# Three-stage order for attention pairs, mask in VectorE's maximum pass, features off GpSimd

## What is computed

```python
B, H, S, D = 4, 8, 576, 64
scores = q @ k.T / 8                      # causal: -1e9 above the diagonal
a = exp(scores - max) ; a /= a.sum + 1e-9
local = a @ v
phi(x) = where(x > 0, x, exp(x) - 1) + 1
mem_out = (phi(q) @ M_prev) / (phi(q) @ z_prev + 1e-6)
g = sigmoid(beta)                         # one per head
x = g * mem_out + (1 - g) * local         # 2304 tokens x 512
# first layer: h = x @ w_in (512 -> 1024); u = h * softmax(h); layer norm with g_ln; @ w_out
# second layer: (sigmoid(x @ w_gate) * (x @ w_val)) @ w_out, width 1536
```

## Time and profile before

| | us |
|---|---|
| median of 3 runs | 964.6 (963.66 to 966.36) |
| profiled execution | 962.04 |
| its span | 960.3 |
| busy PE, DVE, ACT, POOL | 907.2, 408.5, 329.8, 183.5 |
| mean granted TensorE clock | 0.979 |

### The profile page before, as it was taken

How to read it: one execution, slowest core, us unless ns; L and a number is a source line. 1 busy time by engine, 2 the same in 40 slices (tenths; PEclk the granted TensorE clock), 3 DMA queues, 4 the chain that set the end, 5 groups by cost and what they waited for, 6 DMA issues and landing times.

```text
span 960.3 us, 15231 instructions
## 1 busy us (share of the span) xinstructions
PE 907.2 (94%) x5584; PEld 749.3 (78%) x5584; DVE 408.5 (43%) x972; ACT 329.8 (34%) x740; POOL 183.5 (19%) x144
## 2 busy tenths in 40 slices
PE   5787789999999999999799999999999999999997
PEld 2555557777777777878699989989998998998997
DVE  5666776666766676354414422122112112112112
ACT  3455545545554555345524211121112112112111
POOL 4344322222222120125407410010001001001000
PEclk9889999999999999999999999999999999999999
DMA  5131111111111100400305000000000000000000
GB/s 155 49 127 41 51 40 38 31 33 38 38 38 38 38 26 14 132 1 1 99 1 165 0 33 1 1 18 15 0 0 33 0 0 33 0 0 33 0 0 33
DMA packets 36786, 33.51 MB, mean 35 GB/s; under 512 B 5776, under 2 KB 27280, under 8 KB 36752
## 3 DMA queue, kind: packets, MB, share of 16 engines
q1 hardware_dynamic: 36752, 33.06, 11.6%
HBM read 28.33 MB, written 4.72 MB: 34 GB/s over the span
## 4 chain that ended last, share of the span: by engine, by line
PE 87%; DVE 5%; issue 2%; POOL 2%; ACT 1%; DMA 1%; POOLq 0%; ACTq 0%; SPq 0%; DVEq 0%
PE m_bk L1066 8%; PE s_bk L1089 6%; PE tt_bk L1174 5%; PE s_bk L1176 5%; PE s_bk L1174 5%; PE s_bk L1175 5%; PE tt_bk L1176 5%; PE tt_bk L1175 5%; PE o_bk L1007 5%; PE tt_bk L999 4%; PE s_bk L953 4%; PE o_bk L1089 4%; PE m_bk L1191 3%; PE m_bk L1190 3%; PE m_bk L1189 3%; PE s_bk L1066 2%
## 5 line engine op out<-in xcount | busy, mean ns | idle before, releaser
L886 DVE TENSOR_TENSOR gv<-gv,s_bk 128x384 f32<-128x384 f32 x71 | 39.4, 554 | 289.4 <-PE s_bk L1176 289.4
L530 ACT ACTIVATE p_nat<-s_bk,negmax 128x512 f32<-128x512 f32 (+2 forms) x144 | 77.9, 548 | 94.9 <-DVE negmax L729 94.8
L597 ACT ACTIVATE gv<-tt_bk 128x384 f32<-128x384 f32 x70 | 34.5, 492 | 206.7 <-PE tt_bk L1176 206.7
L1174 PE MATMUL tt_bk<-x_hi,w_hi 128*128 128x384 f32 x280 | 94.7, 338 | 8.2 <-POOL x_lo L492 8.2
L1174 PE MATMUL s_bk<-x_hi,w_hi 128*128 128x384 f32 x288 | 96.3, 334 | 0.0
L1176 PE MATMUL s_bk<-x_hi,w_lo 128*128 128x384 f32 x288 | 96.2, 334 | 0.0
L1175 PE MATMUL s_bk<-x_lo,w_hi 128*128 128x384 f32 x288 | 96.2, 334 | 0.0
L1176 PE MATMUL tt_bk<-x_hi,w_lo 128*128 128x384 f32 x280 | 94.3, 337 | 0.0
L1175 PE MATMUL tt_bk<-x_lo,w_hi 128*128 128x384 f32 x280 | 94.0, 336 | 0.0
L604 ACT CAST gv_hi<-gv 128x384 fp32r<-128x384 f32 x72 | 36.9, 513 | 158.0 <-PE m_bk L1191 135.9
L729 DVE TENSOR_REDUCE negmax<-s_bk 128x1 f32<-128x512 f32 (+2 forms) x144 | 67.4, 515 | 51.0 <-PE s_bk L953 42.7
(11 more groups left out here) (144 smaller groups left out, 1846.6 us busy)
## 6 DMA issues: line engine op xcount, KB each, us to landing
qkT<-in_q SPq DMA_DIRECT2D x16, 288.0 KB, 2.8
qkT<-in_k SPq DMA_DIRECT2D x16, 288.0 KB, 2.8
out<-o_sb SPq DMA_DIRECT2D x18, 256.0 KB, 2.0
v_raw<-in_v SPq DMA_DIRECT2D x16, 256.0 KB, 2.7
w_raw<-in_moe_w_gate SPq DMA_DIRECT2D x12, 256.0 KB, 4.5
w_raw<-in_moe_w_val SPq DMA_DIRECT2D x12, 256.0 KB, 4.9
w_raw<-in_moe_w_out SPq DMA_DIRECT2D x12, 256.0 KB, 6.0
xT<-in_moe_w_in SPq DMA_DIRECT2D x1, 2048.0 KB, 8.5
```

What stands on the lines that cost most here:

```text
L530: nc.scalar.activation(dst, s_tile(tile), ACT.Exp, bias=negmax[:, n:n + 1], accum_out=den[:, n:n + 1]).then_inc(exp_ok, 1)
L1174: mm(o, w3_hi[f][:, a], x2_hi[:, d, :], start=d == 0, stop=False)
```

## The change

- A pair spreads over three steps: step g does the scores of g, memory and fills of g-1, and the weighting of g-2. `M0` becomes 6, there are 17 steps, and the last has no scores. No loop is left in this part.
- `p_nat` and the buffer of queries and keys exist twice. Loads of q and k are issued one step earlier, v and the memory rows follow in the later step.
- No mask products and no scaled queries. VectorE's maximum is one `tensor_tensor_reduce`: scores plus a float32 mask, times -1/8, written to `p_nat`, and the minimum of it as the negative maximum. ScalarE takes the exponential in place in `p_nat`.
- Score groups wait for `max_ok` and not for `exp_ok`.
- Features: relu and exp on ScalarE straight from q, and min(exp, 1) + relu on VectorE. GpSimd keeps the splits and the power.
- ScalarE copies fills 0, 2, 4, 5, 6, VectorE 1, 3.
- The tail of the weighted rows goes into a bank of its own (`tail_bank`, in `m_bk`), directly behind the main part.
- The tail scores stand late, among the output products. On ScalarE `moe_x(t + 1)` and `feature_exp(g + 1)` stand ahead of `moe_y(t - 1)`.
- The weights' splits move: W1 to steps 1 and 2, W2 to 4 and 5 (two blocks each) and 6 (four).

```diff
-    M0 = HP + 1
+    M0 = HP + 2
-    T_END = LAST - M0
+    T_END = PAIRS - M0
-        W1_AT = {0: (0, 1), 1: (2, 3)}
-        W2_AT = {2: (0, 1, 2), 3: (3, 4, 5), 4: (6, 7)}
+        W1_AT = {1: (0, 1), 2: (2, 3)}
+        W2_AT = {4: (0, 1), 5: (2, 3), 6: (4, 5, 6, 7)}
...
@@ gpsimd @@
+            def step(g):
+                for c in W1_AT.get(g, ()):
+                    split_w1(c)
+                for f in W2_AT.get(g, ()):
+                    split_w2(f)
+                if g >= M0:
+                    rstd(g - M0)
+                if g >= M0 - 1:
+                    split_x(g - M0 + 1)
...
@@ scalar @@
-                nc.scalar.activation(dst, s_tile(tile), ACT.Exp, bias=negmax[:, n:n + 1],
+                nc.scalar.activation(p_tile(g, tile), p_tile(g, tile), ACT.Exp, bias=negmax[:, n:n + 1], scale=-1.0,
                                      accum_out=den[:, n:n + 1]).then_inc(exp_ok, 1)
...
+            def step(g, t):
+                if g < PAIRS:
+                    exp_tile(g, 0)
+                    exp_tile(g, 1)
+                if t:
+                    moe_ln(t - 1)
+                keep_both(g - 2)
+                if g < PAIRS:
+                    for n in range(2, 8):
+                        exp_tile(g, n)
+                if g < LAST:
+                    feature_relu(g + 1)
+                keep_pt(g - 1, 0)
+                moe_exp(t)
+                keep_pt(g - 1, 2)
+                if g < PAIRS:
+                    exp_tile(g, 8)
+                keep_pt(g - 1, 4)
+                moe_square(t)
+                keep_pt(g - 1, 5)
+                keep_pt(g - 1, 6)
+                for f in W2_AT.get(g, ()):
+                    split_w2(f)
+                moe_x(t + 1, x_done(t + 1))
+                if g < LAST:
+                    feature_exp(g + 1)
+                if t:
+                    moe_y(t - 1)
...
@@ vector @@
-                    last = nc.vector.tensor_reduce(negmax[:, c:c + 1], s_tile(tile),
+                    last = nc.vector.tensor_tensor_reduce(out=to, in0=s_tile(tile), in1=m, scale=-SCALE, scalar=3.0e38,
+                                                          op0=ALU.add, op1=ALU.min, accum_out=negmax[:, c:c + 1])
...
+            def feature(g):
+                dve.wait_ge(qrelu_ok, g + 1)
+                dve.wait_ge(qexp_ok, g + 1)
+                wait(dve, mem_ready, 2 * g)
+                nc.vector.scalar_tensor_tensor(out=phi[:, 0:S], in0=qexp[:, :], scalar=1.0, in1=qrelu[:, :], op0=ALU.min,
+                                               op1=ALU.add).then_inc(phi_ok, 1)
...
+            def early_step(g):
                 unit_max(g, 0)
                 unit_max(g, 1)
+                if g:
+                    normalize(g - 1, 1)
+                    normalize(g - 1, 2)
                 unit_max(g, 2)
                 unit_max(g, 3)
+                if g:
+                    scale_memory(g - 1, 0)
+                    scale_memory(g - 1, 1)
+                    keep_pt(g - 1, 1)
                 unit_max(g, 4)
                 unit_max(g, 5)
+                if g:
+                    keep_pt(g - 1, 3)
+                feature(g)
                 unit_max(g, 6)
+                normalize(g, 0)
...
+            def step(g, t):
+                if g < PAIRS:
+                    unit_max(g, 0)
+                    unit_max(g, 1)
+                if t > 1:
+                    moe_store_x(t - 2)
+                normalize(g - 1, 1)
+                if t:
+                    moe_ln_low(t - 1)
+                normalize(g - 1, 2)
+                if g < PAIRS:
+                    unit_max(g, 2)
+                    unit_max(g, 3)
+                scale_memory(g - 1, 0)
+                scale_memory(g - 1, 1)
+                if g < PAIRS:
+                    feature(g)
+                    unit_max(g, 4)
+                    unit_max(g, 5)
+                    normalize(g, 0)
+                moe_max(t)
+                keep_pt(g - 1, 1)
+                moe_rows(t)
+                moe_stats(t)
+                keep_pt(g - 1, 3)
+                if g < PAIRS:
+                    unit_max(g, 6)
+                for f in W2_AT.get(g, ()):
+                    scale_w2(f)
+                moe_var(t)
+                moe_norm(t)
...
@@ tensor @@
+            def early_step(g):
                 scores(g, 0)
+                if g > 1:
+                    weighted(g - 2)
+                scores(g, 1)
+                if g:
+                    memory(g - 1, None)
+                scores(g, 2)
+                if g:
+                    for n in range(5):
+                        turn_p(g - 1, n)
+                scores(g, 3)
+                if g:
+                    turn_p(g - 1, 5)
+                    turn_p(g - 1, 6)
+
+            def step(g, t):
+                if g < PAIRS:
+                    scores(g, 0)
+                if t > 1:
+                    moe_out_t(t - 2)
+                if t:
+                    pe.wait_ge(pt_act_ok, NA * (g - 1))
+                    pe.wait_ge(pt_dve_ok, ND * (g - 1))
                     moe_transpose(t - 1)
+                weighted(g - 2)
+                wait(pe, yt_ok, t - 1)
+                if g < PAIRS:
+                    scores(g, 1)
+                memory(g - 1, t)
+                pe.wait_ge(x_ok, 2 * (g - 1))
+                wait(pe, u_ok, t)
+                moe_hidden(t, 0, 12)
+                if g < PAIRS:
+                    scores(g, 2)
+                moe_hidden(t, 12, 24)
+                turn_p(g - 1, 0)
+                turn_p(g - 1, 1)
+                if t:
+                    if g < PAIRS:
+                        pe.wait_ge(max_ok, NU * g + NU - 1)
+                    moe_out(t - 1, 0, 8)
+                turn_p(g - 1, 2)
+                turn_p(g - 1, 3)
+                if t:
+                    moe_out(t - 1, 8, 12)
+                if g < PAIRS:
+                    scores(g, 3)
+                if t:
+                    moe_out(t - 1, 12, 16)
+                turn_p(g - 1, 4)
+                turn_p(g - 1, 5)
+                if t:
+                    moe_out(t - 1, 16, 20)
+                turn_p(g - 1, 6)
+                if t:
+                    moe_out(t - 1, 20, 24)
```

More of the change, by code:

```diff
@@ L427, in feature_min @@
[L427 to L435, removed]
+            nc.gpsimd.affine_select(out=mask[:, (FULL - 1) * P:FULL * P], in_=mask[:, (FULL - 1) * P:FULL * P],
+                                    compare_op=ALU.is_ge, fill=MASK, base=0, pattern=[[-1, P]],
+                                    channel_multiplier=1).then_inc(mask_ok, 1)
@@ L454, in rstd, with step @@
                 nc.gpsimd.tensor_tensor(st[:, 6:7], st[:, 5:6], half[:, :], ALU.pow).then_inc(rstd_ok, 1)
[L456 to L483, removed]
+            def step(g):
+                for c in W1_AT.get(g, ()):
[6 more added lines that the diff above has]
+                    split_x(g - M0 + 1)
+            for g in range(PAIRS + 1):
+                step(g)
             def split_w3(f):
@@ L604, in keep_gv_hi, with keep_both @@
                 nc.scalar.copy(gv_hi[f % 2][:, :], gv[f % 2][:, :]).then_inc(gv_hi_ok, 1)
[L606 removed]
+            def keep_both(h):
+                keep_x(h, 0)
+                keep_x(h, 1)
+            def early_step(g):
                 exp_tile(g, 0)
                 exp_tile(g, 1)
[L610 to L619 removed]
+                if g > 1:
+                    keep_both(g - 2)
+                for n in range(2, 6):
+                    exp_tile(g, n)
+                if g:
+                    keep_pt(g - 1, 0)
+                    keep_pt(g - 1, 2)
@@ L866, in _ @@
             dve.wait_ge(gates, 2)
-            feature_relu(0)
             for g in range(M0):
-                step(g, early=W2_AT.get(g, ()))
-            step(M0, t=0, first=True, t_turned=False)
-            step(M0 + 1, t=1, t_turned=False)
-            with dve.Fori(M0 + 2, LAST) as g:
-                step(g, t=g - M0)
-            step(LAST, after=False, t=T_END)
+                early_step(g)
+            for g in range(M0, PAIRS + 1):
+                step(g, g - M0)
             t = T_END
@@ L971, in scores @@
                     for pair in zip(*units):
[L972 to L973 removed]
                         for tile, unit in zip(pair, units):
[L975 removed]
+                            last = score_tile(g, tile)
                             if tile == unit[-1]:
@@ L1138, in _ @@
+            pe.wait_ge(consts, 4)
             pe.wait_ge(zeros, 2)
             for g in range(M0):
-                step(g, before=g > 0)
-            step(M0, t=0, first=True)
-            step(M0 + 1, t=1, turned=False)
-            with pe.Fori(M0 + 2, LAST) as g:
-                step(g, t=g - M0)
-            step(LAST, t=T_END)
+                early_step(g)
+            for g in range(M0, PAIRS + 1):
+                step(g, g - M0)
             t = T_END
-            weighted_main(LAST)
+            weighted(LAST)
```

345 lines of the change are left out of this document (124 added, 221 removed).

## The result

The changed kernel takes 959.0 us (median of 6 runs, 956.3 to 960.6), the kernel before 964.3 us beside it. The ratio is 0.994, with a 95% interval of 0.992 to 0.996: faster, by 5.3 us, where 12.4 us were forecast. The profiled execution's span fell from 960.3 to 957.0 us, by 3.3 us only: the profiled execution of the kernel before lies 2.3 us under its median, that of the changed kernel 0.3 us.

What follows compares the result with a forecast made beforehand. Early steps were taken as held by waits for exponentials and transpose copies, full steps by TensorE's work. Terms of 91 + 55 + 205.1 + 22.1 = 373.2 against 385.6 gave -12.4 us: 952 on the runs' scale, range 939 to 965.

Steps and rivals of the forecast that it cites:

- rival B: Full steps: ScalarE's output copy comes in time, steps run at TensorE's 24.7 us, kernel 944 us; chance 0.17.
- The early steps: Attention-only steps before the first feed-forward tile: that tile's pair starts at 91 us instead of 107.4, a gain of 16.4.
- The walk of one round: Early steps, one tail maximum's end to the next, added up engine by engine: 14.2 us, 5.4 less than before.
- Splitting the layers' weights adds 1.3: Early steps: 1.3 us added to the four rounds' 56.8 us for splitting the layers' weights.
- The 2 us put down for the low clock: Early steps: 2 us added to the four rounds' sum for low-clock stretches.
- The transition: Steps 6 and 7: GpSimd's splits delay its power, TensorE idles some 8 us; both steps take 55 us against 49.2.
- Full steps, TensorE: Full steps: TensorE loses 0.74 us of mask products, leaving 24.7 us of work; moving groups costs nothing visible.
- Full steps, ScalarE: Full steps: the output copy stands last in ScalarE's queue, TensorE waits 0.9 us, a step takes 25.6 us.
- VectorE's edits: Masked maximum costs as before plus up to 0.08 us per tile; features' sum on VectorE costs 0.7 us.
- Rival D: VectorE becomes the bound: masked maximum takes twice the time per column, 3.3 us more per step, 971 us; chance 0.09.
- Rival C: Early steps hardly shrink: waits for memory, transposes and copies plus low clock, rounds 16.8 us, kernel 965; chance 0.17.
- A: The prediction's own sum for the whole kernel: 952 us, alone 945 to 959; chance 0.57.

Runs made afterwards that it cites:

- e5: Changed kernel with GpSimd's four passes over the first weights held back until VectorE's fourth unit of maxima of the next step; 949.4 us (ratio 0.985).
- e8: Changed kernel with the edits of e3, e4 and e5, holding back both weights' splits, low part of x ahead of them; 933.8 us (ratio 0.969).
- e3: Changed kernel with GpSimd's power of a tile issued ahead of the splits of the second weights in step 6; 951.4 us (ratio 0.987).
- e1: Changed kernel with the low parts of the first weights subtracted on VectorE, not on GpSimd; 953.8 us (ratio 0.990).
- e2: Changed kernel with each of GpSimd's four 1024-column passes over the first weights cut into four of 256 columns; 954.4 us (ratio 0.991).
- e6: Changed kernel with two more GpSimd passes in step 4, into buffers that nothing reads; 963.6 us in one run.
- e4: Changed kernel with ScalarE's copy of the layer's output ahead of the next tile's copy and the features' exponential; 952.4 us (ratio 0.988).
- e7: Kernel before with the mask part alone: no mask products, masks in VectorE's maximum pass, exponential from SBUF, full-step loop written out; 953.8 us (ratio 0.990).

## Why the prediction was right and wrong

The direction and the range held; the size did not. 12.4 us were forecast, 5.3 came (3.3 by the two profiled executions, which the table compares). By stretches:

| | forecast | measured | |
|---|---|---|---|
| start of step 6 | 91 | 103.9 | +12.9 |
| steps 6 and 7 | 55 | 55.95 | +1.0 |
| full steps, eight | 8 x 25.6 | 8 x 25.05 | -4.7 |
| step 16 | 22.1 | 21.6 | -0.5 |
| behind the pairs | 574.7 | 575.2 | +0.5 |

That the range held is in part luck: 5 us that the later steps took less than forecast hid part of the 12.9 us of the early ones. Two sums are slightly off: eight steps of 25.6 us are 204.8 and not 205.1, and rival B with early rounds at 13.5 us gives some 941 and not 939. Neither changes the outcome.

**The early steps: the step that failed.** The walk of one round was nearly right: 14.2 us forecast, 14.70 measured in step 4, and 15.0 in step 1 against 15.5. What failed is the term "Splitting the layers' weights adds 1.3". The text gives no working and no row for it, and in the whole walk of the early steps GpSimd's passes have no price: work on an engine that nobody waits for was put at nothing, without a reason. Measured against step 4, step 2 is 4.85 us longer, step 3 6.8 and step 5 2.9, 14.5 us together, where the terms for the splits and the low clock had 3.3. VectorE standing beside GpSimd's passes is 10.3 of the 14.5; the rest goes with the lower clock of these steps. When e5 and e8 moved GpSimd's passes, 13.1 of the 14.5 went: 10.2 in steps 2 and 3, and 2.9 in step 5. The split between the steps differs from execution to execution. From tail maximum to tail maximum, steps 2 and 3 take 19.6 and 21.0 us here, and 20.6 and 20.7 in e3, whose edit does not touch them.

e1, e2, e5 and e6 show the cause: a GpSimd pass with its inputs in SBUF, and a VectorE scaling in SBUF or a pass with two SBUF inputs, exclude each other, whole instruction by whole instruction. The Trainium skill, SBUF — State Buffer, section Who interferes with whom, states this rule: a VectorE pass in a two-port mode, or one with two SBUF inputs against a GpSimd pass that reads SBUF, and the GpSimd pass block each other for the whole instruction. The traces agree: 2.39 us for a scaling and 2.32 for the pass over three numbers in the changed kernel, and in e3 an unchanged 0.69 for the 512-column maximum, which has only one input in SBUF. That the scalings run in a two-port mode is not shown by a run here.

GpSimd's work was not new. New is that the change moved nine scalings from the middle and the end of a step to its start, where GpSimd begins as soon as ScalarE has given it the high parts. In the order before, at this place stood maxima out of PSUM and one relu. That relu carries the mark. By the same count VectorE stood for 4.0 us in all five early steps of the kernel before. The row of the relu:

```profile
L737 DVE TENSOR_SCALAR qrelu<-qkT x16: 445/451/1864, 6.7 to 337.8; 128x576 f32<-128x576 f32 x16
```

A pass that takes 0.45 us took up to 1.86. That one ran from 29.32 to 31.18 us, beside two splits of 2.4 and 2.6 us. Had the walk charged the full length of such splits, the term would have been near 5 us per step.

The 2 us put down for the low clock were about right for what is left when the exclusion is gone (1.4 in step 3 of e5). In the changed kernel step 3 has 2 us more than step 2 at a mean clock of 0.76 against 0.83, and e1, without the exclusion, has two equal steps at 0.90. Whether the stall lets the clock fall stays open. The clock is also low without any stall: 0.89 in step 4 of e1 and of e4, which takes 15.9 us there. And step 6 of the changed kernel keeps 1.00 although VectorE stood for 2.8 us in it, with more products for TensorE in that step.

**The transition.** Forecast some 8 us of idle time before the transposes of step 7, measured 8.37, with the chain as described; without it the step takes 27.5 us (e3). This came from reading the order of one short queue line by line.

**Full steps, TensorE.** 24.7 us of work forecast, 24.24 measured. The mask products were sized right. Missing were the 0.17 of the products that now run as one group (e7), and some 0.25 for the new order, which the text called "nothing visible": both without masks and without waits, a full step takes 24.55 us in the old order (e7) and 24.30 in the new one (e4). That fewer changes between kinds of products are the reason is not shown.

**Full steps, ScalarE.** A wait of 0.9 us was forecast, with its cause, and 0.81 measured. e4 took it away by the order of three instructions. Rival B, full steps of 24.7 us because the copy comes in time, did not come: the wait was there, and the step's 25.05 us lie near 24.7 only because TensorE's own work was less than forecast.

**VectorE's edits.** The maximum with mask costs what the maximum cost, 0.68 us for 512 columns. The first line is the kernel before, the others the changed one:

```profile
L729 DVE TENSOR_REDUCE negmax<-s_bk 128x1 f32<-128x512 f32 x16 | 10.3, 686 | 5.9 <-PE s_bk L953 5.9
...
L719 DVE CUSTOM_DVE_ANT_0 p_nat<-s_bk,mask 128x512 f32<-128x512 f32 x12 | 7.8, 684 | 0.0
...
L727 DVE SCALAR_TENSOR_TENSOR phi<-qexp,qrelu 128x576 f32<-128x576 f32 x6 | 4.5, 748 | 0.0
```

Rival D falls. The features' sum took 0.75 us (0.7 forecast). The rule of the Trainium skill, Vector Engine (DVE) Microarchitecture Reference, section Points that are easy to get wrong, that such a pass with two SBUF sources wider than bf16 runs at half throughput, is not seen here: the prediction's estimate by it was 1.3.

**Rival C** gave the early rounds 16.8 us and 965 us in all. The low clock it named did occur (0.83, 0.76, 1.00 and 0.90 in steps 2 to 5), but the waits for memory, transposes and copies do not fill the rounds: step 4 has them all and takes 14.70 us. The lengths that came (19.55, 21.45, 14.70, 17.6) have the exclusion as their main cause. C came about as near in size as A (6 us off against 7), for a wrong reason.

So two waits that the change itself brought in took 6.5 and 7 us, and the exclusion, with what the clock lost beside it, some 13 us, out of a gain that would else have been some 30; e8 shows 29.9. The forecast had both waits and not the third.

## What to carry to other kernels

When an order is changed, ask of each VectorE pass that is moved not only who waits for it, but what GpSimd does at its new place. The maximum among an instruction's durations, beside its median, shows an exclusion that no table of waits names; here that table had only TensorE waiting for VectorE. And after a regrouping, read the last instructions of each in-order queue: here three instructions' order on ScalarE and two on GpSimd were worth 14 us.

## What was not expected of the hardware

- The wait for GpSimd is independent of the VectorE pass's size: a pass over three numbers per partition, 0.16 us by itself, stood 2.32 us.
- GpSimd waits as well: a split of 512 columns that began while a VectorE scaling ran took 1.73 us in e3, where the others take 1.26 to 1.39. Cutting its work costs more than that waiting: eight pieces took 5.99 us, of which some 5.6 without any wait, the same columns in two pieces 4.82.
- The fused maximum with its accumulator read costs the chain nothing beyond the plain reduce: the second 512-column pass begins 0.61 to 0.62 us after the first in both kernels' timelines.
